# Local and dilated attention with a top-2 adapter on one core: the loads of batches 2 to 6 as six runs per partition in place of three

## The reference

```python
scores = (1 / sqrt(D)) * q @ k.transpose(0, 1, 3, 2)
mask_plain = (rel >= 0) & (rel < 32)
mask_dil = (rel >= 0) & (rel < 128) & (rel % 4 == 0)
attn = softmax(where(mask, scores, -1e9))
x = (attn @ v) as [B * S, H * D]
logits = x @ w_gate
topk = the two largest of 8
delta[token] += w[token, k] * ((x[token] @ A[e]) @ B[e])
out = x + delta
```

## Time and profile before

| what | value |
|---|---|
| median of 3 runs | 100.47 us (100.41 to 103.09) |
| profiled execution | span 99.2 us (from its first to its last instruction; the page gives no other time for it) |
| median less span | 1.3 us |
| busy: TensorE, weight loads, VectorE, ScalarE, GpSimd | 81.6, 59.9, 62.3, 71.0, 54.6 us |
| granted TensorE clock | 0.981 of full speed |
| moved by DMA | 24.50 MB in 5807 packets |

### The profile page before, as it was taken

The page is one execution under the profiler, slowest core; times in us unless marked ns, Lnnn a source line. Parts: engine busy times, 40 slices in busy tenths (PEclk is TensorE's granted clock), DMA queues, the critical chain, the costliest instruction groups (busy, mean ns, idle before and its releaser), DMA issues.

```text
span 99.2 us, 3611 instructions
## 1 busy us (share of the span) xinstructions
PE 81.6 (82%) x1587; PEld 59.9 (60%) x1587; DVE 62.3 (63%) x138; ACT 71.0 (72%) x123; POOL 54.6 (55%) x73
## 2 busy tenths in 40 slices
PE   3999969959569989999897979999799989766200
PEld 2443457548356765779676859878687878545100
DVE  5770007706468189359746697779676999979700
ACT  5195494399938983896997679989689899757200
POOL 5999900880549136404942297099085574637800
PEclk9999999999999999999999999999999999999975
DMA  2999999999999999999999999999979988979991
GB/s 33 300 204 208 207 214 226 201 217 220 211 211 211 214 219 213 219 216 206 210 217 212 224 212 214 210 204 175 198 264 412 415 353 360 426 297 401 420 422 76
DMA packets 5807, 24.50 MB, mean 247 GB/s; under 512 B 800, under 2 KB 928, under 8 KB 5024
## 3 DMA queue, kind: packets, MB, share of 16 engines
q0 software_dynamic: 3920, 14.23, 71.9%
q1 hardware_dynamic: 1728, 9.77, 23.9%
q10 hardware_dynamic: 144, 0.28, 1.0%
HBM read 29.07 MB, written 9.44 MB: 388 GB/s over the span
## 4 chain that ended last, share of the span: by engine, by line
PE 57%; ACT 18%; DVE 9%; DMA 5%; issue 3%; POOL 2%; POOLq 0%
PE ps L213 49%; ACT p L351 11%; PE ps L414 5%; DMA out_dram<-x 5%; DVE x L551 4%; DVE x L390 3%; ACT xt L424 2%; PE ps L504 1%; ACT zs L472 1%; POOL x L559 1%; ACT in L263 1%; POOL xb L397 1%; PE ps L438 1%; ACT xt L427 1%; DVE top L492 1%
## 5 line engine op out<-in xcount | busy, mean ns | idle before, releaser
L397 POOL CAST xb<-x 128x1152 bf16<-128x1152 f32 (+1 forms) x16 | 18.3, 1144 | 25.4 <-DVE x L390 25.4
L351 ACT ACTIVATE p<-ps 128x960 bf16<-128x960 f32 (+1 forms) x32 | 27.6, 899 | 4.2 <-PE ps L213 4.1
L213 PE MATMUL ps<-in,p 128*64 128x130 bf16 (+1 forms) x416 | 21.5, 221 | 3.7 <-ACT p L351 3.1
L390 DVE TENSOR_TENSOR x<-ps,rec 128x1152 f32<-128x1152 f32 x16 | 21.7, 1358 | 0.5
L213 PEld LDWEIGHTS ps<-in,p 128*64 128x64 bf16 (+1 forms) x416 | 17.1, 104 | 7.2 <-ACT p L351 4.1
L551 DVE TENSOR_TENSOR x<-x,ps 128x1024 f32<-128x1024 f32 (+1 forms) x16 | 17.5, 1116 | 3.4 <-PE ps L213 3.4
L387 DVE RECIPROCAL rec<-ps 128x18 f32<-128x18 f32 x16 | 4.3, 270 | 17.5 <-PE ps L213 17.3
L213 PE MATMUL ps<-warm 128*128 128x512 f32 x22 | 13.1, 737 | 1.5 <-DVE warm L217 1.5
L499 POOL TENSOR_TENSOR gz<-zs,g 128x640 bf16<-128x640 f32 x7 | 8.9, 1275 | 9.4 <-DVE g L494 9.4
L213 PEld LDWEIGHTS ps<-in 64*64 64x64 bf16 x576 | 10.9, 106 | 2.9 <-issue 0.9
L213 PE MATMUL ps<-in 64*64 64x96 bf16 (+1 forms) x576 | 11.9, 201 | 0.7 <-issue 0.7
(11 more groups left out here) (55 smaller groups left out, 101.8 us busy)
## 6 DMA issues: line engine op xcount, KB each, us to landing
out_dram<-x SPq DMA_DIRECT2D x6, 1152.0 KB, 6.1
in<-in_qkv_dram POOLq DMA_DIRECT2D x5, 1152.0 KB, 22.1
in<-in_qkv_dram POOLq DMA_DIRECT2D x10, 292.5 KB, 23.1
in<-in_qkv_dram POOLq DMA_DIRECT2D x10, 288.0 KB, 8.2
out_dram<-x SPq DMA_DIRECT2D x4, 576.0 KB, 3.8
in<-in_qkv_dram POOLq DMA_DIRECT2D x10, 146.2 KB, 8.1
in<-in_qkv_dram POOLq DMA_DIRECT2D x2, 434.2 KB, 13.7
awf<-in_aw_dram ACTq DMA_DIRECT2D x1, 272.0 KB, 3.8
```

Source lines behind the costliest of these rows:

```text
L213: return nc.tensor.matmul(o, lhsT=lhsT, rhs=rhs, start=start, stop=stop, skip_group_check=True)
L351: return [nc.scalar.activation(p[:, :, :].rearrange("p h (s c) -> p h s c", c=PER)[:, :, b0 : b0 + nb, 0:SEG], PS[:, k.at : k.at + 2, 0 : ...
L390: nm = add(f"N{tag}", "DVE", ("el", XG), lambda: [nc.vector.tensor_tensor(X[r][:, XG * g : XG * g + XG].rearrange("p (b i n) -> p b i n", ...
L397: add(f"B{tag}", "POOL", ("el", cut), lambda: [nc.gpsimd.tensor_copy(XB[r % 2][:, g, 0:cut], X[r][:, XG * g : XG * g + cut])], [nm] + free)
```

## The change

In the host's array the two QK runs of batches 2 to 6 become four of HQK = 1152 elements, with 16 elements between them, and the run of 2 VB becomes two of VB with 16 elements between them. The two load forms of L301 and L305 get one dimension more; the destination is the same. Each of the three DMAs of a batch moves the same bytes to the same place as before. Batches 0, 1 and 7, the plan, and the order and the waits of all instructions on every engine are as before.

```diff
+HQK = 2 * S
...
             a = add(f"L{r}", "POOL", ("dma", 128, 8 * QK, 1), lambda: [nc.gpsimd.dma_start(
-                out=IN[r % SLOTS][:, 2 * VB : 2 * VB + 2 * QK].rearrange("p (j n) -> p j n", j=2),
-                in_=qkv[r].rearrange("a p n -> (a p) n")[:, 0 : 2 * (QK + PAD)].rearrange("p (j n) -> p j n", j=2)[:, :, 0:QK],
+                out=IN[r % SLOTS][:, 2 * VB : 2 * VB + 2 * QK].rearrange("p (j n) -> p j n", j=4),
+                in_=qkv[r].rearrange("a p n -> (a p) n")[:, 0 : 4 * (HQK + PAD)].rearrange("p (j n) -> p j n", j=4)[:, :, 0:HQK],
             )], [d for d in free if d[0] == "S"])
             b = add(f"Lw{r}", "POOL", ("dma", 128, 8 * VB, 2), lambda: [nc.gpsimd.dma_start(
-                out=IN[r % SLOTS][half(h), ROW * h : ROW * h + 2 * VB],
-                in_=qkv[r, h, :, 2 * (QK + PAD) : 2 * (QK + PAD) + 2 * VB],
+                out=IN[r % SLOTS][half(h), ROW * h : ROW * h + 2 * VB].rearrange("p (j n) -> p j n", j=2),
+                in_=qkv[r, h, :, 4 * (HQK + PAD) : 4 * (HQK + PAD) + 2 * (VB + PAD)].rearrange("p (j n) -> p j n", j=2)[:, :, 0:VB],
             ) for h in range(2)], [d for d in free if d[0] == "V"])
...
-    whole = np.zeros((B, 2, 64, ROW + 3 * PAD), a.dtype)
+    whole = np.zeros((B, 2, 64, ROW + 6 * PAD), a.dtype)
...
-                whole[r, h, :, g * (QK + PAD) :][:, :QK] = a[r, h, :, x : x + QK]
-            whole[r, h, :, 2 * (QK + PAD) :][:, : 2 * VB] = a[r, h, :, y : y + 2 * VB]
+                for i in range(2):
+                    whole[r, h, :, (2 * g + i) * (HQK + PAD) :][:, :HQK] = a[r, h, :, x + HQK * i : x + HQK * i + HQK]
+            for i in range(2):
+                whole[r, h, :, 4 * (HQK + PAD) + i * (VB + PAD) :][:, :VB] = a[r, h, :, y + VB * i : y + VB * i + VB]
```

## The result

22 runs of each kernel: 101.31 us median with six runs per partition, 100.90 with three. The ratio is 1.005, 95% interval 1.0032 to 1.0068: half a microsecond slower, small but clear of noise. The profiled execution of the changed kernel took 101.33 us, its span is 99.5 us (99.2 before). Wherever an execution has both numbers on record, the device time is 1.7 to 1.9 us over the span, so the profile of before belongs to an execution of about 101.0 us, somewhat over its median.

What follows compares the result with a forecast made beforehand. Loads start the stores; row 5's store, set by compute or the store chain, plus a fixed 10.5 us ends the kernel. Stream +0.5 us, less cover, gave +0.2 us; span 99.4 + 1.3 = 100.7 us, range 99.8 to 102.2.

Steps and rivals of the forecast that it cites:

- the signs that the prediction set for itself: Checks including row 5's store at 88.1 waiting for row 3's landing, not GpSimd, and a 10.5 us tail after it.
- What a packet costs: Load queue, batches 2 to 6: 4 ns per added packet, 120 per DMA engine, so 0.5 us on the stream.
- the windows: Two spans of the load queue in the trace before, 10.4 to 12.4 and 22 to 26 us, counted for packet cost.
- The upper bound from the records' lengths: Load queue: by the packet records' own lengths, 31 ns more per split, 3.7 us on the stream.
- Who feels it: Matmuls have 1.5 to 2.7 us of cover and don't wait; the first store moves 72.4 to 72.9, the end +0.2.
- GpSimd's issues: Descriptor writing on GpSimd: 1.3 ns per run, 0.5 us per row; 0.13 us on TensorE, not added to the sum.
- The step that failed: Kernel end: row 5's store issue plus a fixed 10.5 us; compute at 87.8 sets that issue, store chain 0.3 us behind.
- The level: Whole kernel: 1.3 us for what lies around the profiled span, added to 99.4 to give 100.7 us.
- Record-length cost: Rival, load queue: packets cost what their records say, stream 3.7 us longer, time 103.9 us; chance 0.08.
- blocked GpSimd: Rival: GpSimd stands at row 3's loads on a full descriptor queue, TensorE 3.5 us late, time 104.0 us; chance 0.05.
- Sooner fetches: Rival: smaller load packets let instruction fetches through up to 167 ns sooner, time 100.1 us; chance 0.10.
- No split: Rival: runs are merged on the way, packet count stays 3920, time 100.5 us; chance 0.15 together with no cost.

Runs made afterwards that it cites:

- e2: Kernel before with two runs per partition in batches 2 to 6 in place of three; ratio to before 1.000.
- e1: Kernel before with twelve runs per partition in batches 2 to 6 in place of three; ratio to before 1.0135.
- e9: Kernel before, three runs per partition, but the first store also waits for the last two values loads of batch 7; ratio to before 1.0151.
- e11: Changed kernel, six runs per partition, but the first store waits only for batch 7's query and key loads; ratio to the kernel before 0.9988.
- e10: Kernel before, three runs per partition, but the first store waits only for batch 7's query and key loads; ratio to before 1.0019.
- e8: Kernel before, but a whole store waits for the store three before it in place of two; ratio to before 0.9998.
- e3: Kernel before with only batch 6 split into six runs per partition, batches 2 to 5 left at three; single time 101.21 us.
- e4: Kernel before with batches 2 to 5 split into six runs per partition, batch 6 left at three; single time 100.69 us.
- e12: Kernel before with twelve runs per partition in batches 2 to 6 and the first store waiting only for batch 7's query and key loads; ratio 1.0097.
- e5: Kernel before, unchanged with three runs per partition, executed and profiled again; single time 102.97 us.
- e7: Kernel before with twelve runs per partition in batches 2 to 6, as in e1, executed and profiled again; single time 102.98 us.

## Why the prediction was right or wrong

The forecast was 100.7 against 100.5, +0.2 us within 99.8 to 102.2; measured is +0.5% on a level of 100.9. The time is in the range and the sign is right; the size was under half of what came. By the signs that the prediction set for itself it was wrong in two places: row 5's store waited for GpSimd's addition (87.96) and not for row 3's landing (87.7), and the tail behind it took 10.7 us and not 10.5. That a sum with the wrong tail came out on the right side is in part luck.

- *What a packet costs.* Right, though 4 ns was only the middle of the 0 to 7.8 that the windows left open; the periods give 3.9. The stream was forecast 0.5 us longer; the first store went out 0.43 later. Row 3's landing moved from 87.5 to 87.7, not to 88.0. The upper bound from the records' lengths, 3.7 us, had nothing to do with the cost.
- *Who feels it.* No matmul was late for a load of batches 2 to 7 in the profile after, but the cover was thinner than forecast, since TensorE happened to be early: batch 6's scores began at 63.35 against a landing at 61.9, 1.5 us in place of 2.7, and batch 7's at 71.41 against 71.2, 0.2 in place of 1.5. The loads that TensorE did wait for, 1.0 us in all, were those of batch 1.
- *GpSimd's issues.* The slope was wrong. An issue over 128 partitions took 608, 787, 821 and 965 ns with 128 (e2), 256, 512 and 1024 (e1) runs, so the 1.3 ns per run, taken between two DMAs of different shape, doesn't hold within one shape; the step that the change makes is 34 ns, not 0.33 us. Over 64 partitions it was some 70 ns for 64 runs more. Together 0.2 us per batch, not 0.5.
- *The step that failed* is the end: "the issue of row 5's store plus a fixed 10.5 us", with "compute set it, with the store chain only some 0.3 us behind". The tail isn't fixed. It is 9.8 us if row 3's store has landed early enough and up to 10.9 if not; then the end is row 3's landing plus 11.0. With 9.8, the profile of before would have ended at 97.7; it ended at 98.4 = 87.5 + 11.0 (rounded). So in that execution the store chain already set the end, by 0.7 us, and a delay of row 3's landing had no 0.3 us of cover to get through. In the sum, the term at the end was +0.2 for a landing 0.5 later, through an issue 0.2 later; in the profiles the landing is 0.26 later and the end 0.27. e9 (later start, 1.5% slower) and e11 (earlier start, cost gone) show that the cost goes this way. Its size isn't accounted for: the profiles have 0.3 of some 0.5 us, e9's profile has 0.5 of 1.5, and e10 and e8 gained nothing, which doesn't fit a store chain that sets the end by 0.7 us in most executions.
- *A part that the forecast didn't have.* The addition before row 5's store ended at 87.73 to 87.90 in the profiles at full clock with two or three runs, at 87.96, 88.38 and 88.48 with six, and at 89.05 and 88.92 with twelve. Some of it shows up as TensorE's unreleased stops: 1.8, 1.9, 1.8 and 2.3 us for two or three runs; 2.3, 3.1 and 2.1 for six; 3.8 and 2.7 for twelve. (The mixed ones, e3 and e4, have 2.5 and 2.6.) An earlier start of TensorE also goes with longer stops (e10), but among the profiles at full clock in which it starts at 10.3 to 10.6 us (before, e9; e11; e12) it is still 1.8 and 1.8, 2.1, and 2.7, with the addition at 87.83 and 87.85, 88.48, and 88.92. e5 against e7 (90.47 and 90.50) doesn't have it. So compute that gets later with more packets is an untested rival for a part of the cost, of twelve runs above all, and why the stops get longer is open. Each begins 0.6 to 2.0 us after an instruction fetch has started and ends 1.2 to 1.6 us after the fetch's packet has ended, so they look like waits for instructions. That load packets delay a fetch isn't shown: from its start to TensorE's going on it was 2.2 to 2.5 us with two or three runs, 2.2 to 2.7 with six, 2.2 to 2.5 with twelve.
- *The level.* The 1.3 us for what lies around the span came from a profile and a median of different executions; within one execution it is some 1.8. As it was in both sums, it changes nothing in the difference.
- *Rivals.* Record-length cost and blocked GpSimd: excluded by e1. Sooner fetches: not seen, since the times from fetch to going on are no shorter with shorter packets, and the kernel didn't get faster. No split: 5840 packets.

## What to carry to other kernels

The load stream of this kernel paid 3.5 to 3.9 ns of each engine's time for a packet, so count the packets per engine and multiply; read the cost from how many packets pass in a window, not from their recorded lengths, which overlap. Then look for what the end of the stream starts: a few tenths of a microsecond on loads that had cover against all their own readers still reached the end, because the first store waited for the last loads. And when two paths end within half a microsecond of each other, compare the whole of both to the last landing, not to the last instruction that they share.

## What was not expected

- The per-packet cost was the same, 3.5 to 3.9 ns, from 9216 B to 1152 B packets, while the queue's share by its records rose from 71.7% to 80.1%.
- In each of the three profiles with an unreleased stop of TensorE of 1.65 to 1.70 us (e5, e7, e8) the granted clock was 0.50 for 3.4 us, from within 0.8 us of the end of that stop; after stops of 1.42 and 1.55 us (e1) it stayed at 1.00. The executions of e5 and e7 took 103.0 us, 2.3 us over the median of the kernel before beside them, that of e8 101.93.
- An instruction fetch of 16 KB took 0.88 to 1.5 us on its DMA engine, and where TensorE stood still at one, it went on 2.2 to 2.7 us after the fetch began, whatever size the load packets had.
